# The opening of an attention stage: centroid norms in a chain of their own, similarities by thirds, another order around the second head

## The chip, the cores and the metric

The kernel runs on one core of one Trainium2 chip. The metric is the device time of one launch, in microseconds (us). A core has a matrix engine (TensorE, PE in the profile, with its weight loads as PEld), a vector engine (VectorE, DVE), a scalar engine (ScalarE, ACT), a general engine (GpSimd, POOL) and a sync engine (SyncE, SP) that here only issues DMA transfers. Each engine takes its own instructions strictly in the order in which they are written, and waits on semaphores for the others. ACT can issue DMA transfers as well; they then have their own queue.

## What is computed

An attention with clusters, followed by two expert layers. Only the attention's opening is touched.

```python
q_n = q / (np.linalg.norm(q, axis=-1, keepdims=True) + 1e-06)
k_n = k / (np.linalg.norm(k, axis=-1, keepdims=True) + 1e-06)
c_n = centroids / (np.linalg.norm(centroids, axis=-1, keepdims=True) + 1e-06)
q_assign = np.argmax(np.einsum('bhsd,hcd->bhsc', q_n, c_n), axis=-1)
k_assign = np.argmax(np.einsum('bhsd,hcd->bhsc', k_n, c_n), axis=-1)
mask = q_assign[:, :, :, None] == k_assign[:, :, None, :]
scores = np.where(mask, scale * np.matmul(q, k.transpose(0, 1, 3, 2)), -1000000000.0)
...
x = _moe_ref(x=x, **moe_kwargs)
return _moe2_ref(x=x, **moe2_kwargs)
```

There are 2 batches and 8 heads, so 16 pairs of batch and head (called heads here), each with 768 tokens of 64 numbers, and 16 centroids a head. The first expert layer norms its 8 expert embeddings of 512 numbers (`en = expert_emb / norm`) and divides by a number tau; the kernel folds those embeddings into a small matrix while attention still opens.

## The kernel before

A head's queries and keys come as six tiles each of 128 tokens. PE transposes the 12 tiles in three groups of four (`transpose_raw`): tiles 0 to 3 are queries, 4 and 5 queries and 6 and 7 keys, 8 to 11 keys. Every group is then split into a high part by ACT (`prep` stages 0, 1 and 2, semaphore `prep_hi`) and a low part by DVE (the same stages, semaphore `prep_lo`, one count for each group, so that the first head's groups are 1 to 3 and the second head's 4 to 6). `similarities` multiplies the 12 tiles with the 16 centroids of the head, two matmuls of 16 columns for a tile (L369 and L370 for queries, L372 and L373 for keys). DVE takes the maximum over the 16 and turns it into a cluster number (`prep` stage 4: L665, L667, L638, L676); the keys' numbers go into a small tile (`attn_key_id_b`, L770), PE spreads them over all partitions (`key_ids`, L379), and ACT copies that out (L559, semaphore `kid_ready`).

Attention itself goes by query tiles n = 0, 1, 2 and so on. PE makes `scores` (four matmuls of 384 columns, L417 and L418), DVE compares cluster numbers (`mask`, L685) and adds the mask while it takes the row maximum (`maxima`, L697, semaphore `max_done`), ACT makes the exponentials (L564), PE transposes them (L428), ACT and DVE split the transposed tile (L570 and L643, `attn_probs_t_hi` and `attn_probs_t_lo`), PE multiplies with the values (L447). `step(0)` is the first step of the regular pipeline, in which scores run three tiles ahead. Two score banks are used in turn, so `scores(2)` needs the maximum of tile 0 taken.

Ahead of that pipeline stands an opening that is written out by hand, engine by engine, and it is this that the change rewrites:

- `UnitRows` norms the centroids (128 rows of 64) and the expert embeddings (8 rows of 512) together. DVE squares and sums both, ACT takes one square root over both columns (L149), DVE refines it with six small operations (`newton`) and writes the unit centroids (L169, two operations); the unit embeddings are written much later (L169 again), just ahead of the first mask.
- PE transposes the unit centroids (L504), ACT (L608, L609) and DVE (L643 on `attn_c_lo` and `attn_c_hi_over_lo`) split them.
- `warm(n)` issues n matmuls of 512 columns on constants whose result nobody reads; `WARM` holds their numbers, in the order in which they are called.
- PE transposes the 8 heads' unit embeddings (L525, semaphore `experts_t`); DVE scales them by 1/tau into `fold` (L784, semaphore `x_done`), ahead of its third `maxima`.

ACT needs a table for square roots and another for exponentials, and loads one when it changes (ACT_TABLE_LOAD).

## Time and profile before

| what | us |
|---|---|
| median of 3 runs | 1592.2 |
| lowest and highest of them | 1591.24 and 1592.25 |
| the profiled execution, its own time | 1594.29 |
| its span, first to last instruction | 1592.5 |
| PE busy in it | 1568.3 (98%) |
| DVE busy | 1190.0 (75%) |
| ACT busy | 770.6 (48%) |

The views used are the page (engines' busy time, the chain of waits), the timeline of the opening (each row one instruction or a run of like ones, with the idle time ahead of it and what ended that) and windows (busy time of each engine in a stretch, the clock granted to TensorE as a share of full, the DMA engines' share and rate). Attention takes about the first 480 us of the span, and its opening the first 25 us.

### The profile page before, as it was taken

The page shows a single profiled execution, that of the slowest core. Times are in us where ns is not written, and L with a number is a line of the kernel's source. Part 1 is how long each engine was busy: PE and PEld are TensorE (multiplying, and loading weights), DVE is VectorE, ACT ScalarE, POOL GpSimd, SP SyncE. Part 2 cuts the span into 40 slices and gives each one's busy share as a digit, 9 for nine tenths or more (in the row PEclk, how much of TensorE's full clock was granted, in tenths as well). Part 3 has the DMA queues.
Part 4 walks back from the last instruction along what each step waited for, and adds up shares of the span by engine and source line. Part 5 has one row for each costly group of instructions (what it writes and reads, how often), then busy time and mean ns, then how long its engine had stood idle before and what let it go on. Part 6 is the DMA issues. An engine that isn't in the chain of part 4 may idle for free.

```text
span 1592.5 us, 27473 instructions
## 1 busy us (share of the span) xinstructions
PE 1568.3 (98%) x8404; PEld 1390.7 (87%) x8404; DVE 1190.0 (75%) x2026; ACT 770.6 (48%) x1418; POOL 263.7 (17%) x343
## 2 busy tenths in 40 slices
PE   8999999999999999999999999999999999999998
PEld 7999999778888788989999898989899998989897
DVE  7999999999999976876656666666656566666664
ACT  5777779888888852323232323233232333232321
POOL 2111111342333550000100100010001001100102
PEclk9999999999999999999999999999999999999999
DMA  4222323354344310100110010011001100100002
GB/s 101 61 60 69 79 59 90 86 198 148 143 151 151 106 41 27 40 28 27 47 33 27 29 51 27 27 40 40 27 27 45 35 27 28 52 26 27 27 0 79
DMA packets 123701, 94.92 MB, mean 60 GB/s; under 512 B 66345, under 2 KB 101161, under 8 KB 123633
## 3 DMA queue, kind: packets, MB, share of 16 engines
q1 hardware_dynamic: 120848, 86.01, 17.8%
q0 software_dynamic: 2480, 8.13, 1.5%
q8 instruction: 21, 0.34, 0.1%
q14 instruction: 48, 0.39, 0.1%
q10 hardware_dynamic: 304, 0.05, 0.0%
HBM read 87.88 MB, written 6.29 MB: 59 GB/s over the span
## 4 chain that ended last, share of the span: by engine, by line
PE 88%; DVE 7%; issue 3%; ACT 2%; DVEq 0%; DMA 0%; ACTq 0%; POOL 0%
PE moe_bank L1381 11%; PE moe_bank L1383 11%; PE moe_bank L1382 11%; PE moe_bank L1356 10%; PE moe_bank L1359 10%; PE moe_bank L1358 10%; PE attn_ps_out L447 3%; PE attn_ps_probs_t L428 2%; PE moe_bank L1316 2%; PE moe_bank L1318 2%; PE moe_bank L1317 2%; PE moe_bank L1299 2%; PE moe_bank L1301 2%; PE moe_bank L1300 2%; DVE attn_scores L697 1%
## 5 line engine op out<-in xcount | busy, mean ns | idle before, releaser
L2035 DVE SCALAR_TENSOR_TENSOR all_x<-moe_bank,all_x 128x512 f32<-128x512 f32 x336 | 251.4, 749 | 130.8 <-PE moe_bank L1383 130.2
L1356 PE MATMUL moe_bank<-moe_x_t_hi,all_w_hi 128*128 128x384 f32 x896 | 303.0, 338 | 2.0 <-DVE all_w_lo L889 1.4
L1359 PE MATMUL moe_bank<-moe_x_t_hi,all_w_lo 128*128 128x384 f32 x896 | 302.5, 338 | 0.0
L1381 PE MATMUL moe_bank<-moe_w_hi,moe_h_hi 128*128 128x512 f32 x768 | 302.3, 394 | 0.0
L1358 PE MATMUL moe_bank<-moe_x_t_lo,all_w_hi 128*128 128x384 f32 x896 | 301.1, 336 | 0.0
L1382 PE MATMUL moe_bank<-moe_w_lo,moe_h_hi 128*128 128x512 f32 x768 | 300.5, 391 | 0.0
L1383 PE MATMUL moe_bank<-moe_w_hi,moe_h_lo 128*128 128x512 f32 x672 | 264.5, 394 | 0.0
L1356 PEld LDWEIGHTS moe_bank<-moe_x_t_hi,all_w_hi 128*128 128x128 f32 x896 | 168.4, 188 | 13.4 <-issue 2.0
L1358 PEld LDWEIGHTS moe_bank<-moe_x_t_lo,all_w_hi 128*128 128x128 f32 x896 | 168.4, 188 | 10.0
L1359 PEld LDWEIGHTS moe_bank<-moe_x_t_hi,all_w_lo 128*128 128x128 f32 x896 | 168.2, 188 | 0.0
L2196 POOL TENSOR_TENSOR moe_w_sums<-moe_dense_w_raw 128x256 f32<-128x256 f32 x32 | 24.8, 774 | 842.4 <-DVE all_w_lo L889 842.4
L1382 PEld LDWEIGHTS moe_bank<-moe_w_lo,moe_h_hi 128*128 128x128 f32 x768 | 144.1, 188 | 23.0
L1381 PEld LDWEIGHTS moe_bank<-moe_w_hi,moe_h_hi 128*128 128x128 f32 x768 | 144.3, 188 | 21.5
L1383 PEld LDWEIGHTS moe_bank<-moe_w_hi,moe_h_lo 128*128 128x128 f32 x672 | 126.0, 188 | 30.1
L1729 ACT ACTIVATE moe_h_hi<-all_x 128x384 fp32r<-128x384 f32 x63 | 33.1, 525 | 170.4 <-DVE all_x L2147 170.4
L889 DVE TENSOR_TENSOR moe_routed_w_lo<-moe_w_raw,moe_routed_w_hi 128x1024 fp32r<-128x1024 f32 x76 | 112.8, 1524 | 0.1
L1705 ACT ACTIVATE moe_h_hi<-moe_p 128x384 fp32r<-128x384 f32 x63 | 33.1, 525 | 143.2 <-DVE moe_p L2101 143.2
L2101 DVE TENSOR_TENSOR moe_p<-moe_bank,moe_p 128x384 f32<-128x384 f32 x63 | 35.1, 557 | 86.8 <-PE moe_bank L1359 76.1
L643 DVE TENSOR_TENSOR attn_probs_t_lo<-attn_ps_probs_t,attn_probs_t_hi 128x384 fp32r<-128x384 f32 x192 | 97.3, 547 | 2.4 <-ACT attn_probs_t_hi L570 1.3
L1724 ACT ACTIVATE moe_h_hi<-moe_bank 128x384 fp32r<-128x384 f32 x63 | 31.0, 492 | 134.2 <-PE moe_bank L1359 134.2
L697 DVE CUSTOM_DVE_ANT_0 attn_scores<-attn_ps_scores,attn_mask 128x768 f32<-128x768 f32 x96 | 91.2, 950 | 2.5 <-issue 0.6
L564 ACT ACTIVATE attn_probs<-attn_scores,attn_row_max 128x768 f32<-128x768 f32 x96 | 91.4, 952 | 3.4 <-DVE attn_row_max L697 3.3
(339 smaller groups left out, 3071.4 us busy)
## 6 DMA issues: line engine op xcount, KB each, us to landing
all_w_raw<-in_moe_w SPq DMA_DIRECT2D x8, 2048.0 KB, 7.5
moe_w_raw<-in_moe_w SPq DMA_DIRECT2D x8, 2048.0 KB, 8.3
moe_dense_w_raw<-in_moe_w SPq DMA_DIRECT2D x64, 256.0 KB, 2.9
moe_dense_w_raw<-in_moe_w SPq DMA_DIRECT2D x32, 512.0 KB, 3.4
attn_q_raw<-in_q SPq DMA_DIRECT2D x32, 192.0 KB, 3.0
attn_k_raw<-in_k SPq DMA_DIRECT2D x32, 192.0 KB, 3.5
attn_v_raw<-in_v SPq DMA_DIRECT2D x16, 192.0 KB, 3.5
tokens<-all_x SPq DMA_DIRECT2D x32, 96.0 KB, 1.9
```

Of the source, the lines that this page charges most:

```text
L447: mm = pe.matmul(out, V2[j][:, m, :], probs[(s0 // 3) % 2][:, m, :], start=(m == 0 and probs is PTH), stop=(m == T - 1 and probs is PTL))
L564: act.activation(PR[s % 2][:], SM[s % 2][:], ACT.Exp, bias=MX[s % 2][:], scale=-1.0, accum_out=SUM[:, s % 12:s % 12 + 1]).then_inc(exp_don ...
L643: return dve.tensor_tensor(out, src, hi.bitcast(F32), ALU.subtract)
L697: dve.tensor_tensor_reduce(out=SM[s % 2][:].rearrange("p (a k) -> p a k", a=2), in0=ps_s[s % 2][:, :, 0:3 * P], in1=MASK[s % 2][:].rearran ...
L889: return dve.tensor_tensor(out, src, hi.bitcast(F32), ALU.subtract)
L1356: pe.matmul(out, hi[:, s, k, :], XH[chunk][:, x, k, :], start=(start and k == 0), stop=False, skip_group_check=True)
L1358: pe.matmul(out, hi[:, s, k, :], XL[chunk][:, x, k, :], start=False, stop=False, skip_group_check=True)
L1359: mm = pe.matmul(out, lo[:, s, k, :], XH[chunk][:, x, k, :], start=False, stop=(stop and k == 1), skip_group_check=True)
L1381: pe.matmul(out, HH[h][hidden][:, rows], W2H[j][:, f, :], start=(f == 0), stop=False)
L1382: pe.matmul(out, HH[h][hidden][:, rows], W2L[j][:, f, :], start=False, stop=False)
L1383: mm = pe.matmul(out, HL[h][hidden][:, rows], W2H[j][:, f, :], start=False, stop=(f == 1))
L2035: dve.scalar_tensor_tensor(acc, y, PROB[:, row, bass.ds(at, 1)], acc, ALU.mult, ALU.add).then_inc(y_added, 1)
```

## The change

The two norms become two chains. The centroids' chain has its own load (from ACT's queue, as before), sum, root, refinement and write. The embeddings' chain is loaded from SP's queue, its squares are summed by ACT (one activation that also sums), its root is taken by ACT later, its refinement is done by DVE right ahead of the first head's maxima over similarities, and ACT instead of DVE writes the unit embeddings. The first head's keys are loaded from ACT's queue, right behind the centroids, instead of from SP's; tau is loaded from SP's queue behind the second head's transfers. PE transposes the unit centroids ahead of the first keys, and ACT and DVE split them ahead of the second group. The 24 similarity matmuls of the first head come in three groups of 8, each waiting only for its own low part. `scores(0)` and four more matmuls of `warm` go ahead of the second head's transposes; the second head's last group of tiles goes behind the keys' numbers on PE and ACT, and behind the second `maxima` on DVE; `scores(2)` goes ahead of the second head's similarities and the embeddings' transposes.

```diff
-WARM = (8, 4, 6)
+WARM = (8, 4, 4, 6)
...
+        dve.tensor_reduce(self.s[0], self.square[:], AX.X, ALU.add).then_inc(self.summed, 1)
+
+    def sums_of_squares(self, act):
+        act.wait_ge(self.loaded, 16)
+        act.activation(self.square[:], self.raw[:], ACT.Square, accum_out=self.s[0]).then_inc(self.summed, 1)
 
     def roots(self, act):
-        act.wait_ge(self.step, self.SUMS)
-        act.activation(self.s[:, 1, :], self.s[:, 0, :], ACT.Sqrt).then_inc(self.root, 1)
+        act.wait_ge(self.summed, 1)
+        act.activation(self.s[1], self.s[0], ACT.Sqrt).then_inc(self.root, 1)
 
     def scale(self, dve):
-        s, step = self.s, self.step
-        dve.memset(s[:], 1.0).then_inc(step, 1)
-        for j, (rows, _) in enumerate(self.arrays):
-            raw, square = self.raw[j], self.square[j]
-            dve.wait_ge(self.loaded[j], 16)
-            dve.tensor_tensor(square[:], raw[:], raw[:], ALU.mult).then_inc(step, 1)
-            dve.wait_ge(step, 2 + 2 * j)
-            dve.tensor_reduce(s[0:rows.shape[0], 0, j:j + 1], square[:], AX.X, ALU.add).then_inc(step, 1)
         dve.wait_ge(self.root, 1)
-
-        newton(dve, step, self.SUMS, s[:, 0, :], s[:, 1, :], s[:, 2, :], s[:, 3, :])
-        dve.wait_ge(step, self.SUMS + 6)
-
-    def write(self, dve, j):
-        rows, outs = self.arrays[j]
-        for out in outs:
-            raw = self.raw[j][:].rearrange("r (h d) -> r h d", d=DH) if len(out.shape) == 3 else self.raw[j][:]
-            dve.tensor_scalar(out, raw, self.s[0:rows.shape[0], 2, j:j + 1], None, ALU.mult).then_inc(self.step, 1)
+        newton(dve, self.step, 0, *self.s)
+
+    def outputs(self):
+        for out in self.outs:
+            yield out, self.raw[:].rearrange("r (h d) -> r h d", d=DH) if len(out.shape) == 3 else self.raw[:]
+
+    def write(self, dve):
+        dve.wait_ge(self.step, self.SCALED)
+        for out, raw in self.outputs():
+            dve.tensor_scalar(out, raw, self.s[2], None, ALU.mult).then_inc(self.written, 1)
+
+    def write_by_scalar(self, act):
+        act.wait_ge(self.step, self.SCALED)
+        for out, raw in self.outputs():
+            act.activation(out, raw, ACT.Copy, scale=self.s[2]).then_inc(self.written, 1)
...
+        cents = UnitRows(mem, "centroids", centroids.rearrange("h c d -> (h c) d"), [unit[:, 0], unit[:, 1]])
+        embeddings = UnitRows(mem, "embeddings", expert_emb, [unit_experts[:, :, 0, :], unit_experts[:, :, 1, :]])
...
             for half in range(2):
                 sp.dma_start(QR[0][:, :, half, :], qd[0:1].rearrange("o p t d -> p (o t) d")).then_inc(first_q, 16)
-            for half in range(2):
-                sp.dma_start(KR[0][:, :, half, :], kd[0:1].rearrange("o p t d -> p (o t) d")).then_inc(first_k, 16)
             sp.dma_start(VR[0][:], vd[0:1].rearrange("o p t d -> p (o t) d")).then_inc(first_v, 16)
+            embeddings.load(sp)
             load(1, 1)
+            sp.dma_start(TAU[:, 0:1], tau.rearrange("(o n) -> o n", o=1).broadcast_to([P, 1])).then_inc(tau_loaded, 16)
             load_next(2, 0)
             load_next(3, 1)
...
-                    warm(WARM[2], ps_o[:])
+                    warm(WARM[3], ps_o[:])
...
             pe.wait_ge(first_q, 32)
             transpose_raw(0, 0, 4).then_inc(prep_ready, 1)
             transpose_raw(0, 4, 2, ps_t[:, 0], 4)
+            pe.wait_ge(cents.written, 2)
+            pe.transpose(ps_o[:, 0:P], unit[:].rearrange("p o d -> p (o d)"), c["ident"][:]).then_inc(cent_ready, 1)
             pe.wait_ge(first_k, 32)
             transpose_raw(0, 6, 2, ps_t[:, 0], 4).then_inc(prep_ready, 1)
             transpose_raw(0, 8, 4, ps_t[:, 1]).then_inc(prep_ready, 1)
-            pe.wait_ge(rows.step, rows.FIRST)
-            pe.transpose(ps_o[:, 0:P], unit[:].rearrange("p o d -> p (o d)"), c["ident"][:]).then_inc(cent_ready, 1)
             warm(WARM[1])
             pe.wait_ge(cent_split, 4)
-            pe.wait_ge(prep_lo, 3)
-            similarities(0, 0, ps_o[:, P:P + 2 * T * NC], 0)
-            similarities(0, 0, ps_o[:, P:P + 2 * T * NC], T).then_inc(prep_ready, 1)
+            for first in range(0, 2 * T, 4):
+                pe.wait_ge(prep_lo, first // 4 + 1)
+                mm = similarities(0, 0, ps_o[:, P:P + 2 * T * NC], first, 4)
+            mm.then_inc(prep_ready, 1)
+            scores(0, 0, 0)
+            warm(WARM[2], ps_s[1][:, 1])
             pe.wait_ge(raw_loaded[1], LOADS)
             transpose_raw(1, 0, 4, ps_s[1][:, 0]).then_inc(prep_ready, 1)
             transpose_raw(1, 4, 4, ps_s[1][:, 1]).then_inc(prep_ready, 1)
-            transpose_raw(1, 8, 4, ps_t[:, 1]).then_inc(prep_ready, 1)
-            scores(0, 0, 0)
             pe.wait_ge(idb_ready, 1)
             key_ids(ps_t[:, 0], 0)
             key_ids(ps_p[:], 3)
+            transpose_raw(1, 8, 4, ps_t[:, 1]).then_inc(prep_ready, 1)
             pe.wait_ge(prep_lo, 5)
             scores(1, 1, 0)
+            pe.wait_ge(max_done, 1)
+            scores(2, 2, 0)
             pe.wait_ge(kid_ready, 2)
             pe.wait_ge(prep_lo, 6)
             similarities(1, 1, ps_p[:], 0)
-            pe.wait_ge(rows.step, rows.DONE)
+            pe.wait_ge(embeddings.written, 2)
             for h in range(H):
                 mm = pe.transpose(ps_o[:, h * E:(h + 1) * E], unit_experts[:, h].rearrange("e o d -> e (o d)"),
                                   c["ident"][0:E, 0:E])
             mm.then_inc(experts_t, 1)
-            pe.wait_ge(max_done, 1)
-            scores(2, 2, 0)
...
-            rows.load(act)
-            act.dma_start(TAU[:, 0:1], tau.rearrange("(o n) -> o n", o=1).broadcast_to([P, 1])).then_inc(tau_loaded, 16)
-            rows.roots(act)
-            act.wait_ge(made, 4)
-            act.activation(TABLE[:], c["rank16"][:, 0:1], ACT.Exp)
+            cents.load(act)
+            for half in range(2):
+                act.dma_start(KR[0][:, :, half, :], kd[0:1].rearrange("o p t d -> p (o t) d")).then_inc(first_k, 16)
+            cents.roots(act)
             prep(0, 0, 0)
-            prep(0, 0, 1, ps_t[:, 0])
-            prep(0, 0, 2, ps_t[:, 1])
             act.wait_ge(cent_ready, 1)
             act.activation(CH[:], ps_o[:, 0:P], ACT.Copy).then_inc(cent_split, 1)
             act.activation(CHL[:], ps_o[:, 0:P], ACT.Copy).then_inc(cent_split, 1)
+            prep(0, 0, 1, ps_t[:, 0])
+            prep(0, 0, 2, ps_t[:, 1])
+            embeddings.sums_of_squares(act)
+            embeddings.roots(act)
+            act.wait_ge(made, 4)
+            act.activation(TABLE[:], c["rank16"][:, 0:1], ACT.Exp)
+            embeddings.write_by_scalar(act)
             prep(1, 1, 0, ps_s[1][:, 0], 5)
             prep(1, 1, 1, ps_s[1][:, 1], 6)
-            prep(1, 1, 2, ps_t[:, 1], 7)
-            prep(0, 0, 5, ps_t[:, 0], 8)
-            prep(0, 0, 6, ps_p, 9)
+            prep(0, 0, 5, ps_t[:, 0], 7)
+            prep(0, 0, 6, ps_p, 8)
+            prep(1, 1, 2, ps_t[:, 1], 9)
...
-            rows.scale(dve)
-            rows.write(dve, 0)
+            cents.sums(dve)
+            cents.scale(dve)
+            cents.write(dve)
             prep(0, 0, 0)
-            prep(0, 0, 1, ps_t[:, 0])
-            prep(0, 0, 2, ps_t[:, 1])
             dve.wait_ge(cent_split, 2)
             low(CL[:], ps_o[:, 0:P], CH[:]).then_inc(cent_split, 1)
             low(CHL[DH:P, :], ps_o[DH:P, 0:P], CH[DH:P, :]).then_inc(cent_split, 1)
+            prep(0, 0, 1, ps_t[:, 0])
+            prep(0, 0, 2, ps_t[:, 1])
             dve.wait_ge(made, ALL_MADE)
+            embeddings.scale(dve)
             prep(0, 0, 4, ps_o[:, P:P + 2 * T * NC])
             dve.wait_ge(ids_step, 3)
             dve.tensor_copy(IDB[:], ID[0][:, T:2 * T]).then_inc(idb_ready, 1)
             prep(1, 1, 0, ps_s[1][:, 0])
             prep(1, 1, 1, ps_s[1][:, 1])
-            prep(1, 1, 2, ps_t[:, 1])
-            rows.write(dve, 1)
             mask(0, 0, 0)
             maxima(0, 0)
             mask(1, 1, 0)
             maxima(1, 1)
+            prep(1, 1, 2, ps_t[:, 1])
             mask(2, 2, 0)
```

What stands in a row on three engines, before and after; `attn_qk_hi1` and `attn_q_lo1` are the second head's split tiles, with 64x512 the last group.

DVE around the first mask, before:

```order
L655 SCALAR_TENSOR_TENSOR attn_qk_hi1<-attn_ps_scores1,attn_qk_hi1 64x256
L655 SCALAR_TENSOR_TENSOR attn_qk_hi1<-attn_ps_probs_t,attn_qk_hi1 64x512 [waits attn_prep_hi]
L169 TENSOR_SCALAR attn_unit_experts<-attn_raw1,attn_row_norms 8x8x64 x2
L685 TENSOR_SCALAR attn_mask0<-attn_key_id_rows0,attn_cluster_id0 128x768 [waits attn_kid_ready]
L697 ISA attn_scores0,attn_row_max0<-attn_ps_scores0,attn_mask0 128x768 [waits attn_scores_ready,attn_mask_ready]
L697 ISA attn_row_max0 128x1
L685 TENSOR_SCALAR attn_mask1<-attn_key_id_rows0,attn_cluster_id0 128x768
```

and after:

```order
L668 SCALAR_TENSOR_TENSOR attn_qk_hi1<-attn_ps_scores1,attn_qk_hi1 64x256
L698 TENSOR_SCALAR attn_mask0<-attn_key_id_rows0,attn_cluster_id0 128x768 [waits attn_kid_ready]
L710 ISA attn_scores0,attn_row_max0<-attn_ps_scores0,attn_mask0 128x768 [waits attn_scores_ready,attn_mask_ready]
L710 ISA attn_row_max0 128x1
L698 TENSOR_SCALAR attn_mask1<-attn_key_id_rows0,attn_cluster_id0 128x768
L710 ISA attn_scores1,attn_row_max1<-attn_ps_scores1,attn_mask1 128x768 [waits attn_scores_ready,attn_mask_ready]
L710 ISA attn_row_max1 128x1
L668 SCALAR_TENSOR_TENSOR attn_qk_hi1<-attn_ps_probs_t,attn_qk_hi1 64x512 [waits attn_prep_hi]
```

The last group (64x512) moved from ahead of the first mask to behind the second maxima, and the two writes of unit experts left this engine.

PE from the second head's first transposes on, before:

```order
L343 MATMUL attn_ps_scores1<-all_ident,attn_q_raw1 128x128 [waits attn_raw_loaded1]
L343 MATMUL attn_ps_scores1<-all_ident,attn_q_raw1 128x128 x5
L343 MATMUL attn_ps_scores1<-all_ident,attn_k_raw1 128x128 x2
L343 MATMUL attn_ps_probs_t<-all_ident,attn_k_raw1 128x128 x4
L417 MATMUL attn_ps_scores0<-attn_qk_hi0 128x384
L418 MATMUL attn_ps_scores0<-attn_qk_hi0,attn_q_lo0 128x384
L417 MATMUL attn_ps_scores0<-attn_qk_hi0 128x384
L418 MATMUL attn_ps_scores0<-attn_qk_hi0,attn_q_lo0 128x384
L379 MATMUL attn_ps_probs_t<-all_identb,attn_key_id_b 128x128 [waits attn_key_id_b_ready]
L379 MATMUL attn_ps_probs_t<-all_identb,attn_key_id_b 128x128 x2
L379 MATMUL attn_ps_prep<-all_identb,attn_key_id_b 128x128 x3
```

and after, from the first head's scores:

```order
L424 MATMUL attn_ps_scores0<-attn_qk_hi0 128x384
L425 MATMUL attn_ps_scores0<-attn_qk_hi0,attn_q_lo0 128x384
L424 MATMUL attn_ps_scores0<-attn_qk_hi0 128x384
L425 MATMUL attn_ps_scores0<-attn_qk_hi0,attn_q_lo0 128x384
L499 MATMUL attn_ps_scores1<-all_onesb 128x512 x4
L350 MATMUL attn_ps_scores1<-all_ident,attn_q_raw1 128x128 [waits attn_raw_loaded1]
L350 MATMUL attn_ps_scores1<-all_ident,attn_q_raw1 128x128 x5
L350 MATMUL attn_ps_scores1<-all_ident,attn_k_raw1 128x128 x2
L386 MATMUL attn_ps_probs_t<-all_identb,attn_key_id_b 128x128 [waits attn_key_id_b_ready]
L386 MATMUL attn_ps_probs_t<-all_identb,attn_key_id_b 128x128 x2
L386 MATMUL attn_ps_prep<-all_identb,attn_key_id_b 128x128 x3
L350 MATMUL attn_ps_probs_t<-all_ident,attn_k_raw1 128x128 x4
```

Scores of tile 0 and four constant matmuls now stand ahead of the second head's transposes, and the last four of these behind the keys' numbers.

ACT from its first instructions, before:

```order
L145 DMA attn_raw0<-in_centroids 128x64
L145 DMA attn_raw1<-in_moe_expert_emb 8x512
L600 DMA attn_tau<-in_moe_tau 128x1
L149 ACT_TABLE_LOAD
L149 ACTIVATE attn_row_norms<-attn_row_norms 128x2 [waits attn_rows_step]
L603 ACT_TABLE_LOAD
L603 ACTIVATE attn_exp_of_rank<-all_rank16 128x1 [waits all_const_made]
L549 ACTIVATE attn_qk_hi0<-attn_ps_prep 128x512 [waits attn_prep_ready]
L549 ACTIVATE attn_qk_hi0<-attn_ps_probs_t 128x256 [waits attn_prep_ready]
```

and after:

```order
L144 DMA attn_centroids_raw<-in_centroids 128x64
L610 DMA attn_k_raw0<-in_k 128x6x64 x2
L158 ACT_TABLE_LOAD
L158 ACTIVATE attn_centroids_norms<-attn_centroids_norms 128x1 [waits attn_centroids_summed]
L558 ACTIVATE attn_qk_hi0<-attn_ps_prep 128x512 [waits attn_prep_ready]
L614 ACTIVATE attn_c_hi<-attn_ps_out 128x128 [waits attn_cent_ready]
L615 ACTIVATE attn_c_hi_over_lo<-attn_ps_out 128x128
L558 ACTIVATE attn_qk_hi0<-attn_ps_probs_t 128x256 [waits attn_prep_ready]
L560 ACTIVATE attn_qk_hi0<-attn_ps_probs_t 128x256
L560 ACTIVATE attn_qk_hi0<-attn_ps_probs_t 128x512 [waits attn_prep_ready]
```

The second table load moved behind the first head's copies and two embeddings operations, and the first head's keys are issued ahead of the first table load.

## Rows read from the trace of the kernel before

**Rows 1.** The page: the chain that ended last by engine.

```profile
PE 88%; DVE 7%; issue 3%; ACT 2%; DVEq 0%; DMA 0%; ACTq 0%; POOL 0%
```

**Rows 2.** Windows, regular attention: us from and to, length, busy us (count), clock, DMA, GB/s.

```profile
30.00:60.00 30.00, 29.66 (x210) 27.90 (x209) 29.66 (x73) 24.25 (x57) 3.23 (x5) 1.00 0.30 73
```

**Rows 3.** Timeline, transfers of the opening: start, length, engine, what.

```profile
1.22 0.78 ACTq L145 DMA_DIRECT2D attn_raw<-in_moe_expert_emb  x1
...
2.21 1.33 SPq L318 DMA_DIRECT2D attn_k_raw<-in_k  x2
...
5.35 1.28 ACT L603 ACT_TABLE_LOAD   x1
...
5.47 0.63 PE L343 MATMUL attn_ps_prep<-all_ident,attn_q_raw 128*128 128x128 f32 x4 [0.86 <-POOL all_fold L123]
...
6.72 0.87 PE L343 MATMUL attn_ps_probs_t<-all_ident,attn_k_raw 128*128 128x128 f32 x6 [0.40 <-DMA attn_k_raw<-in_k]
6.75 0.58 ACT L549 ACTIVATE attn_qk_hi<-attn_ps_prep 128x512 fp32r<-128x512 f32 x1
...
7.51 1.15 SPq L293 DMA_DIRECT2D attn_v_raw<-in_v  x1
```

**Rows 4.** Timeline, ACT and DVE: root and end of the centroids' chain, then the splitting.

```profile
5.13 0.20 ACT L149 ACTIVATE attn_row_norms<-attn_row_norms 128x2 f32<-128x2 f32 x1 [1.43 <-DVE attn_row_norms L159]
...
6.57 0.42 DVE L169 TENSOR_SCALAR attn_unit_centroids<-attn_raw,attn_row_norms 128x64 f32<-128x64 f32 x2
...
7.37 0.69 DVE L643 TENSOR_TENSOR attn_q_lo<-attn_ps_prep,attn_qk_hi 128x512 fp32r<-128x512 f32 x1 [0.38 <-ACT attn_qk_hi L549]
...
8.40 1.03 DVE L655 SCALAR_TENSOR_TENSOR attn_qk_hi<-attn_ps_probs_t,attn_qk_hi 64x256 fp32r<-64x256 f32 x2
...
9.79 0.29 DVE L643 TENSOR_TENSOR attn_c_hi_over_lo<-attn_ps_out,attn_c_hi 64x128 fp32r<-64x128 f32 x1
```

**Rows 5.** Timeline, PE: constant matmuls, the second head's transposes, scores of tile 0.

```profile
7.54 1.03 PE L492 MATMUL attn_ps_scores<-all_onesb 128*128 128x512 bf16 x4
...
14.55 1.54 PE L343 MATMUL attn_ps_scores<-all_ident,attn_q_raw 128*128 128x128 f32 x6
...
17.49 0.49 PE L418 MATMUL attn_ps_scores<-attn_qk_hi,attn_q_lo 128*128 128x384 f32 x1
...
17.81 0.34 PE L417 MATMUL attn_ps_scores<-attn_qk_hi 128*128 128x384 f32 x1
```

**Rows 6.** Windows over the opening (columns as in Rows 2), from two answers.

```profile
4.00:6.00 2.00, 1.14 (x8) 0.57 (x7) 1.59 (x6) 0.85 (x2) 1.37 (x6) 1.00 1.12 239
...
8.57:10.14 1.57, 0.00 (x0) 0.00 (x0) 1.45 (x4) 0.13 (x1) 0.30 (x1) 1.00 1.11 251
10.14:10.90 0.76, 0.76 (x7) 0.76 (x7) 0.00 (x0) 0.00 (x0) 0.00 (x0) 1.00 0.62 162
10.90:14.54 3.64, 3.64 (x19) 3.64 (x18) 0.00 (x0) 0.00 (x0) 0.00 (x0) 0.51 1.05 236
```

**Rows 7.** Timeline, DVE and ACT from the first head's maxima to the first mask.

```profile
14.81 0.36 DVE L665 TENSOR_REDUCE attn_sim_max<-attn_ps_out 128x12 f32<-128x192 f32 x1 [4.72 <-PE attn_ps_out L373]
...
18.04 0.69 DVE L655 SCALAR_TENSOR_TENSOR attn_qk_hi<-attn_ps_probs_t,attn_qk_hi 64x512 fp32r<-64x512 f32 x1
...
18.76 0.87 DVE L169 TENSOR_SCALAR attn_unit_experts<-attn_raw,attn_row_norms 8x512 f32<-8x512 f32 x2
...
18.93 0.48 ACT L559 ACTIVATE attn_key_id_rows<-attn_ps_prep 128x384 bf16<-128x384 f32 x1
...
19.56 0.40 DVE L685 TENSOR_SCALAR attn_mask<-attn_key_id_rows,attn_cluster_id 128x768 bf16<-128x768 bf16 x1
```

**Rows 8.** Timeline: what stands between the first mask and regular attention.

```profile
20.91 0.66 PE L525 MATMUL attn_ps_out<-all_ident,attn_unit_experts 8*128 8x8 f32 x8
...
23.44 0.96 DVE L697 CUSTOM_DVE_ANT_0 attn_scores<-attn_ps_scores,attn_mask 128x768 f32<-128x768 f32 x1
...
25.35 0.92 PE L428 MATMUL attn_ps_probs_t<-all_ident,attn_probs 128*128 128x128 f32 x6 [0.30 <-DVE attn_probs_t_lo L643]
```

34 lines of the change are left out of this document (17 added, 17 removed).

## The prediction, made before the changed kernel ran

> **What bounds the kernel now.** I read the page's chain first: 88% of it is PE's work, 7% DVE's [rows 1]. In regular attention PE and DVE are both busy 29.66 of 30 us [rows 2]; neither has room to make good a late start, so what the opening gains or loses reaches the end one for one. The change touches nothing behind the opening. The question is then how much earlier PE enters the regular pipeline. A good mark is PE's second transposes of probabilities, 25.35 in the trace: they waited for DVE's low parts, which follow the third row maximum, started at 23.44 [rows 8]. The time of that third maximum is my meter: everything behind it is the same in both kernels.
>
> Then I read the opening in order of time. PE transposes the first head's queries at 5.47 and the keys at 6.72, each when their transfers have landed [rows 3]. DVE gets its first high part only at 7.37, since ACT was loading its exponential table (5.35, 1.28 long) and copied at 6.75 [rows 3, 4]. DVE then works without a break to 10.1, the centroids' parts last [rows 4]; PE does nothing from 8.57 to 10.14 [rows 6]. Its 24 similarity matmuls run to 14.7: the first 7 at the full level of the clock (0.76 us for 7, 0.11 each), the other 17 at half of it, 1.2 GHz (clock 0.51, 3.64 us for 17, 0.21 each) [rows 6]. DVE's maximum starts at 14.81, its first mask at 19.56 [rows 7].
>
> **Up to the similarities: 3.5 us earlier.** ACT now issues two key transfers ahead of its square root table. A pair cost SP 1.33 [rows 3]; from 1.22 on that ends at 2.6, the table load of 1.28 at 3.9, and the root no longer waits for the embeddings (it stood at 5.13). From root to unit centroids it is 6.99 less 5.13, 1.86 [rows 4], so they are ready at 5.8, under the query transposes; these end at 6.3, then the centroids' transpose takes 0.1. The exponential table is out of the way: ACT copies at 6.1 instead of 6.75, DVE starts at 6.75 instead of 7.37. Its five splitting operations still take 2.7 together, but the two for the centroids are second and third: done by 8.0. PE has the keys at 6.72 as before (taken unchanged: the DMA engines are full from 4 to 6 us, share 1.12 [rows 6], so an earlier issue brings little; if it brought the whole 1.0 us the following would be 0.4 us earlier, the bound on that side). Its six transposes end at 7.4, four constant matmuls take 1.0 [rows 5], and at 8.4 instead of 10.14 the first third starts: 1.75 gained. A third is 8 x 0.11 = 0.9; second and third start at 9.3 and 10.2, when their low parts (8.9 and 9.5) are there. The splitting by thirds therefore costs no wait, and PE's own work is the bound. They end near 11.2, with or without a fall of the clock at 10.9 as in the trace. DVE can start at 11.3 instead of 14.81: 3.5 earlier.
>
> The embeddings' six refinement steps stand ahead of that maximum on DVE. Six such steps took 1.2 (5.37 to 6.57, the latter in [rows 4]); DVE is free for them at 9.5, so they end at 10.7, covered by the third third of the similarities; without that cover they would cost 1.2. ACT's square with sum (near 0.7, as its 512 wide copy of 0.58 and an accumulator read), root 0.2, table 1.28 and two writes (0.5 each) lie between 8.1 and 11.8, ahead of the second head's first copy near 13.4: free. Loading tau and the embeddings from SP moves the second head's transfers by 0.6 us at most either way, and v's last one, issued at 7.51 before, lands by 12.0 if it takes the 4.5 us that the first keys took from 2.21 to 6.72 [rows 3]; PE asks at 12.2 or later: free.
>
> **From there to the first mask: 4.1 or 2.6 us earlier.** PE now does scores of tile 0 and four constant matmuls before the second head's transposes. At the full level that is 0.7 + 1.0, and these transposes start at 12.8; at the half level (0.32 for each scores matmul [rows 5], and some 1.7, between 1.0 and 2.0, for the constants) at 14.15; before, at 14.55 [rows 5]. Transposes of the first four tiles 0.65, ACT's three copies 1.03 (an estimate: 0.58 for 512 columns [rows 3] and two of 256 that overlap), its two copies of the keys' numbers 0.38 and 0.49 [rows 7] give 2.6 to the mask with the hops: 15.4 or 16.9, instead of 19.56. Before it was 5.0, as DVE did a last split (0.69) and the unit experts (0.87) ahead of the mask [rows 7]. The keys' numbers are at hand: DVE made them in 1.7 from its maximum, so by 13.0.
>
> **From the first mask to the third maximum: 2.2 us lost.** Before, that was 23.44 less 19.56, 3.9. Now DVE takes mask (0.40) and maximum (0.96) twice, with hops of 0.2 between them (3.0 up to the end of the second), then the split that was moved there (0.69): 3.7. PE stands behind it with the second head's similarities (it waits for that low part), 12 x 0.11 = 1.35, and the embeddings' transposes, 0.66 [rows 8]: 5.7. Only then can DVE write the fold matrix (0.3), and its third maximum is queued behind that: 6.1 instead of 3.9. Behind PE's wait stand the first transposes of probabilities and scores of tile 3. So a stall goes and a new one comes: PE has nothing for 1.4 us after scores of tile 2.
>
> **Sum.** Third maximum at 15.4 + 6.1 = 21.5 (full level) or 23.0 (half level) instead of 23.44: 1.9 or 0.4 us earlier. Nothing says how other executions fall between these levels, so I take the middle, -1.0. The profiled execution was 1594.29 with a span of 1592.5; its likes would be 1593.3 and 1591.5. The median of the runs shown lies 2.1 below the profiled one, 1592.2, and becomes **1591.2**. Taking the bounds of the terms (keys 0.4 earlier; constants dearer by 0.3) this case alone reaches from 1589.5 to 1592.3.
>
> **Rival 1, slower: the clock falls in the new wait.** Before the fall at 10.9, PE had done nothing for 1.57 us and then only 16 column matmuls [rows 6]. The change takes that stretch away but makes another: from the end of scores of tile 2 (mask + 2.4) 1.4 us of nothing, 1.35 us of 16 column matmuls, 0.66 us of 8 column ones. Its likeness speaks for a fall there. Against: the same embeddings' transposes, behind the same similarities but without the idle time, still took 0.66 for eight in the trace [rows 8], at the full level. Price: at half level the next six transposes cost 0.6 more, scores of tile 3 another 0.6, the 12 key similarities 1.25 (0.21 less 0.11 each), and if it lasts over the following step another 1 to 2: 2.5 to 5. I take 3.9 on top of -1.0: +2.9, **1595.1**. It decides from the point at which the fall costs more than the 1.0 gained, which is as soon as it reaches scores of tile 3.
>
> **Rival 2: queries and keys share the DMA engines.** The trace has both on one queue, the queries first, engines full. If two queues take turns, the four transfers of 128 x 384 numbers (0.197 MB each) at 239 GB/s [rows 6] are one stream of 3.3 us, and the queries land near its end, with the keys, 0.8 to 1.1 later than now. PE then has 0.4 more to do after the keys' arrival (the queries' last transposes), as DVE and ACT have slack up to 8.4: -0.6, **1591.6**. If the keys slip too, 1592.1. The Trainium skill states such a rule, in "DMA: Bandwidth & Descriptors", Queues, rings and completion order: each engine goes round robin between the queues it has work for. No row here shows two large transfers on two queues at once.
>
> **Rival 3, faster: the loss behind the mask doesn't come.** If the embeddings' transposes aren't last there (because PE comes to them with time to spare), the 2.2 shrinks to 0.7, the moved split alone: 1592.2 less 3.4 = **1588.8**. Against it stands the written order on PE, so little is left for it. That the thirds or the new order don't act at all is excluded: the order of each engine shows them.
>
> A rule on tables that speaks against this change: "ScalarE: Activation LUTs", What ACT_TABLE_LOAD costs, in the Trainium skill, gives 1.28 us for a load and 1.38 for a drain. By it, the root would come at 5.3 instead of 3.9, the unit centroids at 7.1, and all after it near 0.3 later. The trace disagrees: a load of 1.28 at 5.35 and the next copy of data at 6.75, with a small activation in between [rows 3]. The sum goes by the trace.
>
> **Chances.** Forecast 0.50, rival 1 0.25, rival 2 0.15, rival 3 0.10. A measurement of this kernel can tell about 0.2%, 3.2 us, from no change. Faster by more: rival 3 and a sliver of the forecast, 0.12. Slower by more: nearly half of rival 1 and a little else, 0.14. Within: 0.74. The range leaves out rival 3 and the upper part of rival 1, and takes in 1 us by which runs of one kernel differ: 1588.9 to 1595.9.
>
> **What would show it.** In the changed kernel's timeline: unit centroids before 6; the first similarities near 8.4, all 24 in under 3 us; DVE's first maximum over similarities near 11.3; the first mask between 15.4 and 17; then PE idle until DVE's last split, the fold behind the embeddings' transposes, and the third row maximum about 6.1 behind the first mask. Rival 1 shows as a clock of 0.5 somewhere between 20 and 30 us, rival 2 as query transposes near 6.3, rival 3 as a third maximum within 4.6 of the mask. I am wrong if the second head's transfers, not PE, set the start of its transposes, or if ACT's table or embeddings work runs into the second head's first copy.

## The result, and the profile after

The changed kernel takes 1602.28 us (median of 6 runs, 1598.81 to 1603.0), the kernel before 1592.22 (6 runs). The ratio is 1.0059, with an interval of 1.0046 to 1.0071: it is slower by about 0.6%. I had forecast 1591.2, with 1588.9 to 1595.9 as the range, and slower by over 0.2% at 0.14. That was wrong. The profiled executions lie 7.5 us apart (1601.79 against 1594.29), and 7.1 of those 7.5 can be followed in the opening. The difference of the medians is 10.1, since the profiled execution of before was 2.1 above its own median and that of the changed kernel 0.5 below.

From the page of the changed kernel:

```profile
span 1600.0 us, 27487 instructions
...
PE 1574.1 (98%) x8408; PEld 1393.2 (87%) x8408; DVE 1190.7 (74%) x2027; ACT 773.3 (48%) x1423; POOL 263.5 (16%) x343
...
PE 83%; DVE 9%; issue 5%; ACT 1%; DVEq 1%; DMA 1%; ACTq 0%; POOL 0%
```

The last line is that of [rows 1]: PE's share of the chain fell from 88% to 83%. The timeline of the changed kernel, up to the first mask (start, length, engine, what, and in brackets the idle time ahead and what ended it):

```profile
1.22 1.32 ACTq L610 DMA_DIRECT2D attn_k_raw<-in_k  x2
...
2.58 1.28 ACT L158 ACT_TABLE_LOAD   x1 [2.45 <-issue]
...
3.31 1.24 SPq L300 DMA_DIRECT2D attn_q_raw<-in_q  x2
...
3.87 0.20 ACT L158 ACTIVATE attn_centroids_norms<-attn_centroids_norms 128x1 f32<-128x1 f32 x1
...
6.19 0.63 PE L350 MATMUL attn_ps_prep<-all_ident,attn_q_raw 128*128 128x128 f32 x4 [1.54 <-DMA attn_q_raw<-in_q]
...
7.73 1.54 PE L350 MATMUL attn_ps_probs_t<-all_ident,attn_k_raw 128*128 128x128 f32 x6 [0.58 <-DMA attn_k_raw<-in_k]
...
9.06 1.91 PE L499 MATMUL attn_ps_scores<-all_onesb 128*128 128x512 bf16 x4
...
13.70 0.36 DVE L678 TENSOR_REDUCE attn_sim_max<-attn_ps_out 128x12 f32<-128x192 f32 x1 [1.79 <-PE attn_ps_out L380]
...
19.39 0.42 DVE L698 TENSOR_SCALAR attn_mask<-attn_key_id_rows,attn_cluster_id 128x768 bf16<-128x768 bf16 x1
```

The keys are issued at 1.22 instead of 2.21, and land a whole microsecond later: PE waits for the queries until 6.19 and for the keys until 7.73, where it was 5.47 and 6.72 [rows 3]. (The row at 5.47 puts that wait down to a copy on POOL; the kernel waits there only for constants that were ready long before, and for the queries.) On SP's queue everything behind the queries moved up into the keys' old place: the first head's values are issued at 2.22 instead of 3.59, the second head's queries at 3.31 instead of 4.85. The first maximum over similarities comes at 13.70, 1.1 us sooner than the 14.81 of [rows 7], not 3.5. The first mask comes at 19.39, against 19.56. From there on:

```profile
23.33 0.25 PE L376 MATMUL attn_ps_prep<-attn_c_hi_over_lo,attn_qk_hi 128*128 128x16 f32 x1 [1.33 <-DVE attn_qk_hi L668]
...
24.74 1.02 PE L536 MATMUL attn_ps_out<-all_ident,attn_unit_experts 8*128 8x8 f32 x8
...
25.68 1.54 PE L435 MATMUL attn_ps_probs_t<-all_ident,attn_probs 128*128 128x128 f32 x6
25.87 0.28 DVE L798 TENSOR_SCALAR all_fold<-attn_ps_out,attn_tau 128x64 f32<-128x64 f32 x1 [2.17 <-PE attn_ps_out L536]
26.29 0.96 DVE L710 CUSTOM_DVE_ANT_0 attn_scores<-attn_ps_scores,attn_mask 128x768 f32<-128x768 f32 x1
...
30.72 1.54 PE L435 MATMUL attn_ps_probs_t<-all_ident,attn_probs 128*128 128x128 f32 x6
...
33.34 2.27 PE L499 MATMUL attn_ps_out<-all_onesb 128*128 128x512 bf16 x6
...
38.06 0.82 PE L435 MATMUL attn_ps_probs_t<-all_ident,attn_probs 128*128 128x128 f32 x6
```

and the last of these in the kernel before:

```profile
30.96 0.82 PE L428 MATMUL attn_ps_probs_t<-all_ident,attn_probs 128*128 128x128 f32 x6
```

PE has nothing for 1.33 us until DVE's last low part is done (23.33), and DVE nothing for 2.17 us until the embeddings' transposes are. The third row maximum starts at 26.29 (23.44 before) and the second transposes of probabilities at 30.72 (25.35 before, [rows 8]): 5.4 us late. By the fourth, at 38.06 against 30.96, it is 7.1, and the next two (40.91 and 43.76 against 33.82 and 36.68) are 7.1 late as well. The remaining 0.4 of the profiled executions comes somewhere later and was not followed. Windows of the changed kernel (us from and to, length, busy us of PE, PEld, DVE, ACT and POOL with counts, clock, DMA share, GB/s):

```profile
7.50:10.90 3.40, 3.17 (x12) 2.19 (x12) 2.69 (x7) 2.50 (x9) 1.23 (x2) 0.52 1.30 222
...
14.30:17.70 3.40, 3.40 (x15) 2.41 (x15) 1.16 (x5) 0.60 (x1) 0.00 (x0) 0.53 0.42 97
...
24.60:28.00 3.40, 3.40 (x20) 3.35 (x21) 2.00 (x6) 1.23 (x3) 0.00 (x0) 0.52 0.00 0
28.00:31.40 3.40, 3.40 (x17) 3.40 (x16) 0.98 (x4) 0.67 (x2) 0.00 (x0) 0.50 0.00 0
31.40:34.80 3.40, 3.40 (x13) 2.26 (x12) 3.37 (x8) 1.91 (x4) 2.22 (x7) 0.50 0.01 2
34.80:38.00 3.20, 3.06 (x24) 2.16 (x22) 1.75 (x6) 2.19 (x5) 1.38 (x2) 0.98 0.07 15
```

The clock (third number from the end) was at half, 1.2 GHz, in five of these stretches: 7.5 to 10.9, 14.3 to 17.7, and without a break from 24.6 to 34.8. Before, it was at half only from 10.9 to 17.7, at the similarities and the second head's transposes (0.51 and 0.50 there, 0.98 or more in every stretch up to 38). So both rivals that I had kept apart came together: late transfers in the first 8 us, and a clock that falls behind the new wait.

### The profile page after: what moved, and what is told of

The parts are those of the page before. It is cut to its first block, busy times and chain, and to the rows that moved or that the text cites. A ratio compares the mean times of both kernels' runs of the same rounds, so it can differ in the third digit from the quotient of the medians.

```text
span 1600.0 us, 27487 instructions
## 1 busy us (share of the span) xinstructions
PE 1574.1 (98%) x8408; PEld 1393.2 (87%) x8408; DVE 1190.7 (74%) x2027; ACT 773.3 (48%) x1423; POOL 263.5 (16%) x343
## 3 DMA queue, kind: packets, MB, share of 16 engines
q1 hardware_dynamic: 119440, 85.64, 17.8%
## 4 chain that ended last, share of the span: by engine, by line
PE 83%; DVE 9%; issue 5%; ACT 1%; DVEq 1%; DMA 1%; ACTq 0%; POOL 0%
PE moe_bank L1395 11%; PE moe_bank L1397 11%; PE moe_bank L1396 11%; PE moe_bank L1370 10%; PE moe_bank L1373 10%; PE moe_bank L1372 10%; DVE attn_probs_t_lo L656 2%; PE moe_bank L1330 2%; DVE attn_scores L710 2%; PE moe_bank L1332 2%; PE moe_bank L1331 2%; PE moe_bank L1313 2%; PE moe_bank L1315 2%; PE moe_bank L1314 2%; PE attn_ps_out L454 2%
## 5 line engine op out<-in xcount | busy, mean ns | idle before, releaser
L1395 PEld LDWEIGHTS moe_bank<-moe_w_hi,moe_h_hi 128*128 128x128 f32 x768 | 144.3, 188 | 21.5
L579 ACT ACTIVATE attn_probs_t_hi<-attn_ps_probs_t 128x384 fp32r<-128x384 f32 x192 | 84.2, 495 | 19.5 <-PE attn_ps_probs_t L435 19.1
```

The lines of the kernel that those rows point to most:

```text
L579: act.activation(PTH[(s // 3) % 2][:, 3 * half:3 * half + 3, (s % 3) * P:(s % 3 + 1) * P], ps_t[:, half, 0:3 * P].rearrange("p (m s) -> p ...
L1395: pe.matmul(out, HH[h][hidden][:, rows], W2H[j][:, f, :], start=(f == 0), stop=False)
```

## The experiments

Each edit is against the changed kernel unless it says otherwise. "Fourth transposes" below are PE's fourth transposes of probabilities: 30.96 before, 38.06 in the changed kernel; by then a kernel is in its regular pipeline. Kernels that were measured together share the runs of the kernel before. In the twelve profiled executions, what the fourth transposes are late or early against the kernel before comes back in the time of the launch to within 0.8 us.

### Constant matmuls in the new wait

```diff
             scores(2, 2, 0)
+            warm(6, ps_o[:])
             pe.wait_ge(kid_ready, 2)
```

> The changed kernel with 6 more constant matmuls of 512 columns on PE, behind scores of tile 2 and ahead of the wait for the second head's last low part. They fill the 1.3 us in which PE had nothing (21.9 to 23.3 in the trace of after). Theory 1, the clock: the 7 us of loss at the first repeats of the regular pipeline come from TensorE's clock, which fell to half at 24.6 and stayed there to 34.8 after that idle stretch. With it kept up, the wait itself remains: third row maximum near 25.9, PE's second transposes of probabilities near 28.0 instead of 30.7, and nothing lost behind them, so some 2.7 us over the kernel before: 1595. Theory 2, the wait alone (what stands behind DVE's late split is late, whatever the clock): the time stays at 1602, since the wait is as long as it was, and the constant matmuls can only add up to 0.3.

Measured: 1597.12 (1595.74 to 1597.55), ratio 1.0025 (1.0016 to 1.0035), 5.2 less than the changed kernel and 2 above the 1595 of theory 1. Rows of the timeline of gap_warm, PE:

```profile
21.86 1.47 PE L499 MATMUL attn_ps_out<-all_onesb 128*128 128x512 bf16 x6
...
28.03 0.87 PE L435 MATMUL attn_ps_probs_t<-all_ident,attn_probs 128*128 128x128 f32 x6
```

Windows of the same kernel, over the two stretches that were at half before (columns as above):

```profile
24.60:28.00 3.40, 3.40 (x33) 3.36 (x32) 2.32 (x6) 1.90 (x4) 0.00 (x0) 1.00 0.00 0
28.00:31.40 3.40, 3.33 (x23) 2.32 (x23) 3.32 (x10) 2.18 (x5) 1.57 (x3) 1.00 0.01 2
```

Up to the wait all is as in the changed kernel (first mask 19.41, similarities of the second head at 23.36). Then the clock stays up and the second transposes start at 28.03, as theory 1 had it, the fourth at 33.59. Work that computes nothing, put where PE had nothing to do, gives back 4.5 of the 7.1 us (38.06 less 33.59). The wait alone costs less than its consequence. What is left, 2.6, is the lateness that reached the second transposes.

### Keys from SP's queue again

```diff
+            for half in range(2):
+                sp.dma_start(KR[0][:, :, half, :], kd[0:1].rearrange("o p t d -> p (o t) d")).then_inc(first_k, 16)
             sp.dma_start(VR[0][:], vd[0:1].rearrange("o p t d -> p (o t) d")).then_inc(first_v, 16)
             embeddings.load(sp)
...
             cents.load(act)
-            for half in range(2):
-                act.dma_start(KR[0][:, :, half, :], kd[0:1].rearrange("o p t d -> p (o t) d")).then_inc(first_k, 16)
```

> The changed kernel with the first head's keys loaded from SP's queue again, behind the queries (v, embeddings, the rest behind them). Theory 1, shared DMA engines: two queues made both late; now queries are transposed at 5.5 instead of 6.2 and keys at 6.7 instead of 7.7, the clock stays at full from 7.5 to 10.9, the first similarities start near 8.4 instead of 10.4, and the first mask comes at 15.4 to 17 instead of 19.4. The total gains 2 to 4 us on the changed kernel if the clock behind the mask goes as before, and is 1597 to 1600; by the clock it can also fall elsewhere. Theory 2, the transfers are bound by bandwidth whoever issues them: keys at 7.7 as now, and the total stays at 1602.

Measured: 1599.89 (4 runs, 1595.3 to 1601.21), ratio 1.0044 (1.0027 to 1.006). The timeline of keys_sp:

```profile
5.31 0.67 PE L352 MATMUL attn_ps_prep<-all_ident,attn_q_raw 128*128 128x128 f32 x4 [0.39 <-DMA attn_q_raw<-in_q]
...
6.93 0.88 PE L352 MATMUL attn_ps_probs_t<-all_ident,attn_k_raw 128*128 128x128 f32 x6 [0.62 <-DMA attn_k_raw<-in_k]
...
8.32 0.36 PE L378 MATMUL attn_ps_out<-attn_c_hi_over_lo,attn_qk_hi 128*128 128x16 f32 x1
...
11.28 0.36 DVE L678 TENSOR_REDUCE attn_sim_max<-attn_ps_out 128x12 f32<-128x192 f32 x1 [0.63 <-PE attn_ps_out L382]
...
16.81 0.42 DVE L698 TENSOR_SCALAR attn_mask<-attn_key_id_rows,attn_cluster_id 128x768 bf16<-128x768 bf16 x1
```

Windows of the same kernel (columns as above), where the changed kernel first fell, and ahead of the embeddings:

```profile
7.50:10.90 3.40, 3.40 (x30) 3.01 (x28) 2.67 (x11) 3.34 (x9) 1.51 (x2) 1.00 1.09 228
21.20:24.60 3.40, 3.40 (x26) 3.35 (x26) 1.38 (x4) 0.61 (x2) 0.00 (x0) 0.69 0.02 5
```

Queries and keys are there at 5.31 and 6.93, the similarities start at 8.32, DVE's maximum at 11.28 and the first mask at 16.81. These are the prediction's numbers (8.4, 11.3, and 16.9 at the half level). Theory 1 holds: in these two executions the second queue cost 2.6 us at the first mask, 0.8 of it as later keys and most of the rest through the clock, which was at half from 7.5 on in one and not in the other. But behind the mask the clock fell again, now without the late transfers; so that fall has its own cause. It was at full up to 22.4, at half from 23.0 to 25.5 and at full again from 26.0, behind a wait of 1.34 us like the changed kernel's 1.33. So the same wait can be followed by a long fall or by a short one. This execution, at 1595.3, is the fastest of the four; the others took 1598.95 to 1601.21, and of them no trace was taken.

### DVE's last split one place sooner

```diff
             maxima(0, 0)
+            prep(1, 1, 2, ps_t[:, 1])
             mask(1, 1, 0)
             maxima(1, 1)
-            prep(1, 1, 2, ps_t[:, 1])
```

> The changed kernel with one move on DVE: the second head's last low part behind the first row maximum instead of behind the second. PE's similarities of the second head then wait for nothing once scores of tile 2 are out (21.9), the embeddings' transposes end near 23.9, and the third row maximum starts near 24.5 instead of 26.3. Theory 1 (the idle stretch let the clock fall): with the stretch gone the clock stays at full from 24.6 to 34.8 and the second transposes of probabilities start near 26.6 instead of 30.7: 1593.5 to 1594. Theory 2 (wait alone): 1.8 us less than the changed kernel, 1600.

Measured: 1596.03 (1594.69 to 1600.25), ratio 1.0024 (1.0013 to 1.0034). The timeline of split_early:

```profile
21.40 0.25 PE L376 MATMUL attn_ps_prep<-attn_c_hi_over_lo,attn_qk_hi 128*128 128x16 f32 x1
...
23.40 1.54 PE L435 MATMUL attn_ps_probs_t<-all_ident,attn_probs 128*128 128x128 f32 x6
```

A window of the same kernel (columns as above):

```profile
24.60:28.00 3.40, 3.40 (x21) 3.40 (x20) 1.79 (x6) 1.63 (x4) 0.00 (x0) 0.68 0.00 0
```

The second head's similarities start at 21.40 instead of 23.33, and the first transposes of probabilities at 23.40 instead of 25.68, more than expected, as the first mask came 0.4 sooner in this execution. Theory 1 wanted the clock up afterwards. It was not in this execution: the transposes at 23.40 took 1.54 instead of the 0.82 of the full level, and the window from 24.6 on shows 0.68. Yet the fall was much shorter than the 10.2 us of the changed kernel (at full to 23.0, at full again from 27), with the fourth transposes at 33.22. The median, 6.3 below the changed kernel, is far more than the 1.8 of theory 2. So removing the wait took away most of the loss, but PE had no idle time between scores of tile 2 and this fall: the narrow matmuls can be followed by one without the wait.

### Both: keys from SP, constants in the wait

> Both edits: keys from SP's queue and 6 constant matmuls in the gap. If the two causes are separate, their gains add up: early part at the prediction's times (first mask 15.4 to 17), no fall of the clock behind it, third row maximum at mask plus 6.1, so 21.5 to 23.1, and the total 1590.5 to 1592, no slower than the kernel before. If only one of them is real, it comes out as the better of the two single edits, 1595 or above.

Measured: 1594.09 (1593.21 to 1595.54), ratio 1.0008 (0.9999 to 1.0018). First mask 17.18, fourth transposes 31.35. The gains add up: of the 7.1 us at the fourth transposes 4.5 go with the clock and 2.2 with the keys (33.59 less 31.35), and 0.4 is left. The medians say the same: 5.2 less by the constants alone, 2.4 by the keys alone, 8.2 by both. Where I expected 1590.5 to 1592 it is 2.1 to 3.6 above, so the rest of the change does not bring the 1.0 us forecast: by the medians it is 1.6 behind the kernel before, not clear of no change.

### Both: keys from SP, split sooner

> Both single edits that removed a cause: keys from SP's queue, and DVE's last low part of the second head behind the first row maximum. If PE's queue sets the entry into the regular pipeline (similarities of the second head, embeddings' transposes, then the first transposes of probabilities), then with the first mask at 16.8 to 17.2 the similarities start right behind scores of tile 2, near 19.3, the first transposes of probabilities near 21.5 and the second near 24.2, 1.1 ahead of the kernel before: 1591.3 with the clock at full, and 1593 to 1596 if it falls at 21.2 for one stretch as in the profile of keys_sp. The rival, that DVE's third row maximum sets it, gives that maximum at 22.0 and the same -1.4; the two part in the run with fold late.

Measured: 1594.16 (1592.64 to 1598.12), ratio 1.0015 (1.0004 to 1.0025). In the profiled execution (1592.64) the transposes of probabilities start at 21.50 and 24.17, as expected (21.5, 24.2), with the clock at full from 17.8 on. The opening can be 1.2 us ahead of the kernel before and the median still 0.9 behind it: 3 of the 10 runs took 1597.07 to 1598.12.

### The same without the added constants

```diff
-WARM = (8, 4, 4, 6)
+WARM = (8, 4, 0, 6)
```

> As keys_sp_split_early, without the four constant matmuls ahead of the second head's transposes. They took 1.7 us at half the clock (10.9 to 14.3 was at half in keys_sp). If PE's queue is the bound there, the second head's transposes start at 12.0 to 12.3 instead of 13.3 (the transfers have landed by then), the first mask near 15.6, and the total is 1.2 lower than keys_sp_split_early, 1590 if the clock is given back at 14.3 by the transposes alone. If the constants are what gives it back, the clock stays at half to 17.7, the transposes cost twice, and the total is 1.5 or more higher.

Measured: 1591.91 (1590.25 to 1594.92), ratio 0.9992 (0.9982 to 1.0001). Its timeline:

```profile
11.88 1.49 PE L352 MATMUL attn_ps_scores<-all_ident,attn_q_raw 128*128 128x128 f32 x6
...
15.42 0.42 DVE L698 TENSOR_SCALAR attn_mask<-attn_key_id_rows,attn_cluster_id 128x768 bf16<-128x768 bf16 x1
...
19.87 0.87 PE L437 MATMUL attn_ps_probs_t<-all_ident,attn_probs 128*128 128x128 f32 x6
```

The second head's transposes start at 11.88 instead of 13.51 and the first mask comes at 15.42 instead of 17.05: 1.6 us, the price, mostly at half the clock, of four matmuls that nobody reads. PE's real work alone brought the clock back (at half from 12.0 to 14.8, at full when the scores follow at 15.44; 19.87 took 0.87, the full level). The second transposes of probabilities start at 22.53, 2.8 ahead of the kernel before.

> The same kernel as keys_sp_split_early_nowarm, timed again in more rounds, since its interval against the kernel before touched 1. By PE's second transposes of probabilities (22.5 instead of 25.4) it should be up to 2.8 us faster than the kernel before; the first timing gave 1.3. If the gain is real and only blurred by stretches of half clock elsewhere, 1.5 to 3 us faster, with the interval clear of 1; if it was chance, within 0.7 of it.

Measured again with more runs: 1592.21 (1589.97 to 1594.64, 11 runs) against 1593.33, ratio 0.9993 (0.9984 to 1.0002). Two timings agree on 1.1 to 1.3 us, less than the 1.5 I asked for, and neither interval is clear of 1. The profile of this timing caught another execution of the same program: its first mask came at 15.30, but its transposes of probabilities at 19.84 took 1.54, at half the clock, and the next started at 23.97, 1.4 later than in the other one. From the first mask to those transposes the two executions of one program take 4.45 and 4.54 us; what follows differs by the clock. They are not alike in all: they ran on two chips, and the keys came at 6.78 in one and at 7.30 in the other.

### Two constants where PE was idle for 0.6 us

```diff
+            warm(2, ps_o[:])
             pe.wait_ge(max_done, 1)
             scores(2, 2, 0)
```

against keys_sp_split_early_nowarm.

> keys_sp_split_early_nowarm with two constant matmuls on PE ahead of its wait for the first row maximum, where it was idle for 0.6 us. If some of the executions of the kernel without them lose a stretch of half clock between 17 and 28 (its times spread from 1590.3 to 1594.9), they should spread less here and the median come out 0.5 to 1.5 lower; if the spread comes from elsewhere (the routing at 553 to 560, the end), both have the same median within 0.3.

Measured: 1591.94 (1590.06 to 1592.77, 11 runs), ratio 0.9991 (0.9982 to 1.0). The spread is 2.7 us instead of 4.7, the median only 0.3 lower. The first part of the expectation came out for the spread, the second for the median; eleven runs of each don't show that the spreads differ. Of its profiled execution:

```profile
14.78 0.42 DVE L699 TENSOR_SCALAR attn_mask<-attn_key_id_rows,attn_cluster_id 128x768 bf16<-128x768 bf16 x1
...
19.23 0.87 PE L437 MATMUL attn_ps_probs_t<-all_ident,attn_probs 128*128 128x128 f32 x6
```

This profile is no evidence for the two constants. From the mask to the transposes it takes 4.45 us, as without them, and its mask is 0.6 earlier because the clock was at full from 10.9 to 14.3 (0.60 in the other execution), ahead of the place of the edit. It is the lowest median of the study, 1.4 us under the kernel before, at the limit of what was measured.

### What sets the start of the regular pipeline: the fold matrix moved back

```diff
             mask(2, 2, 0)
+            step(0, 0)
             dve.wait_ge(tau_loaded, 16)
...
-            for s in range(14):
+            for s in range(1, 14):
                 step(0, s)
```

on DVE, against keys_sp_gap_warm.

> keys_sp_gap_warm with DVE's fold matrix (which waits for the embeddings' transposes) moved from ahead of the third row maximum to behind step 0. My prediction took DVE's third maximum, queued behind that wait, as what sets the start of the regular pipeline. If so, the maximum starts near 21.2 instead of 23.7 and the second transposes of probabilities near 24.5 instead of 25.8: 1592.8. The rival: PE's own queue sets it (similarities, embeddings' transposes, transposes of probabilities, scores, 12 key similarities, 2.67 us from first to second transposes of probabilities): then the maximum moves and those transposes stay at 25.8, and the total stays at 1594.1.

Measured: 1594.38 (1592.68 to 1597.51), ratio 1.0007 (0.9997 to 1.0017), as keys_sp_gap_warm. Its timeline, with the first mask, the third row maximum, and the two transposes:

```profile
18.76 0.42 DVE L699 TENSOR_SCALAR attn_mask<-attn_key_id_rows,attn_cluster_id 128x768 bf16<-128x768 bf16 x1
...
23.20 0.96 DVE L711 CUSTOM_DVE_ANT_0 attn_scores<-attn_ps_scores,attn_mask 128x768 f32<-128x768 f32 x1 [0.19 <-DVE attn_mask L699]
...
24.70 0.87 PE L437 MATMUL attn_ps_probs_t<-all_ident,attn_probs 128*128 128x128 f32 x6
...
27.36 0.88 PE L437 MATMUL attn_ps_probs_t<-all_ident,attn_probs 128*128 128x128 f32 x6
```

and the same four in keys_sp_gap_warm:

```profile
17.18 0.42 DVE L699 TENSOR_SCALAR attn_mask<-attn_key_id_rows,attn_cluster_id 128x768 bf16<-128x768 bf16 x1
...
23.11 0.88 PE L437 MATMUL attn_ps_probs_t<-all_ident,attn_probs 128*128 128x128 f32 x6
...
23.71 0.96 DVE L711 CUSTOM_DVE_ANT_0 attn_scores<-attn_ps_scores,attn_mask 128x768 f32<-128x768 f32 x1
...
25.78 0.87 PE L437 MATMUL attn_ps_probs_t<-all_ident,attn_probs 128*128 128x128 f32 x6
```

The two executions differ early on. In this one the queries came at 5.58 against 5.11, and the keys' six transposes at 7.11 took 1.54, the half level (0.87 at 7.03 in the other), though both load the keys from SP's queue; the first mask is 1.6 later for it. (The clock column of the windows shows 1.00 there; the durations tell.) So the distance from the first mask counts. The third row maximum comes at mask + 4.4 instead of mask + 6.5. The transposes of probabilities come at mask + 5.9 and + 8.6 in both. So starting DVE's third maximum 2.1 us sooner moved nothing on PE, and PE's own queue sets the start. The rival holds, and my meter was the wrong one.

### The kernel before, with the keys from ACT's queue

```diff
-            for half in range(2):
-                sp.dma_start(KR[0][:, :, half, :], kd[0:1].rearrange("o p t d -> p (o t) d")).then_inc(first_k, 16)
...
             rows.load(act)
+            for half in range(2):
+                act.dma_start(KR[0][:, :, half, :], kd[0:1].rearrange("o p t d -> p (o t) d")).then_inc(first_k, 16)
```

against the kernel before.

> The kernel before with one part of the change: the first head's keys from ACT's queue, behind centroids and embeddings. Theory 1 (two queues share the DMA engines): queries transposed near 6.2 instead of 5.47 and keys near 7.7 instead of 6.72, and the clock at half from 7.5 to 10.9. The first similarities start near 11.3 instead of 10.1; they then run at the full level to 14.0 instead of 14.7, so the total moves little, 0 to 1.2 us above the kernel before. Theory 2 (the lateness in the changed kernel comes from the centroids' transpose or from the embeddings' transfer ahead of them, not from the queue): queries at 5.4 and keys at 6.7 or sooner, the rest as before.

Measured: 1594.98 (1591.67 to 1596.23), ratio 1.0008 (0.9999 to 1.0018), 1.7 above the kernel before by medians, where at most 1.2 was expected. The timeline of before_keys_act:

```profile
5.68 0.63 PE L341 MATMUL attn_ps_prep<-all_ident,attn_q_raw 128*128 128x128 f32 x4 [0.92 <-DMA attn_q_raw<-in_q]
...
7.95 1.54 PE L341 MATMUL attn_ps_probs_t<-all_ident,attn_k_raw 128*128 128x128 f32 x6 [1.42 <-DMA attn_k_raw<-in_k]
...
14.51 0.36 DVE L665 TENSOR_REDUCE attn_sim_max<-attn_ps_out 128x12 f32<-128x192 f32 x1 [3.01 <-PE attn_ps_out L371]
...
22.50 1.49 PE L426 MATMUL attn_ps_probs_t<-all_ident,attn_probs 128*128 128x128 f32 x6
```

Windows of the same kernel (columns as above):

```profile
7.50:10.90 3.40, 2.95 (x11) 1.93 (x11) 2.18 (x5) 1.68 (x6) 0.71 (x1) 0.56 0.93 228
...
21.20:24.60 3.40, 3.40 (x16) 3.29 (x15) 3.13 (x9) 2.77 (x7) 0.00 (x0) 0.55 0.00 0
```

The keys come at 7.95, 1.2 us later than in the kernel before, and the clock is at half for most of 7.5 to 10.9 (0.56), in a kernel that has nothing else of the change. Theory 1 holds for the keys. The queries came only 0.2 later here, but that does not test how two queues share: the keys are issued at 2.03 here, behind the embeddings, and at 1.22 in the changed kernel, so they had less time beside the queries. Beside the keys stand the transfers that moved up on SP's queue (values at 2.21, the second head's queries at 2.88); how much of the lateness is theirs was not tested. That the embeddings' transfer on SP or the centroids' transpose made the keys late is excluded.

The second window shows something about the other cause. The kernel before has no wait behind the first mask, and here PE was busy without a gap from 19.24 on (12 matmuls of 16 columns, 8 of 8 columns, then scores), yet the clock fell at 21.5 and was back at 25. The keys' lateness had not reached that far: the first mask came at 19.23, 0.3 sooner than in the kernel before. The 0.9 us by which the fourth transposes were late (31.85) arose under that fall. So a fall behind these narrow matmuls does not need the new wait, and the kernel before is open to it too.

## Why the prediction was wrong

**The keys' arrival** was the first step that failed: "PE has the keys at 6.72 as before (taken unchanged...)", with an earlier arrival as the only bound. They came at 7.73. I had the mechanism as rival 2, and priced it at 0.4, with late queries only, and at 0.9 "if the keys slip too". Both were late, and the first mask lost 2.6. What the price left out is the clock: PE was idle for 1.54 and 0.58 us up to the keys, and the clock was at half from 7.5 on, so that the key transposes and four constant matmuls cost 3.2 us (7.73 to 10.9) instead of the 1.7 of the sum. That the idle time let it fall there fits keys_sp (0.39 and 0.62, and full) and before_keys_act (0.92 and 1.42, and half), but fold_late ran these transposes at half with 0.66 and no wait for the keys, so it is likely and not shown. The bound on the dear side was missing: with the engines already full [rows 6], another queue for the keys could only change the order in which transfers are served, and it let later ones (values, the second head's queries) be issued 1.4 and 1.5 us sooner, beside the keys. The prediction had allowed 0.6 at most for that. The keys were late in both kernels that issue them from ACT. The round robin that I cited from the Trainium skill ("DMA: Bandwidth & Descriptors", Queues, rings and completion order) fits that in direction; how evenly the queues took turns no run here shows. Late keys should have stood in the sum, with their price, and not beside it.

**Up to the first mask** the rest of the working was right. With the keys back on SP's queue, the first similarities (8.32), DVE's maximum (11.28) and the first mask (16.81) are the forecast 8.4, 11.3 and 16.9. But 16.9 is the case with the clock at half, and the sum took the middle between it and 15.4. Of the four profiled executions with the keys on SP's queue and the four added constants, three had the mask at 16.8 to 17.2 and fold_late at 18.76; none bore out the middle, which made the forecast 0.6 us too good. The embeddings' steps on DVE, ACT's work on the embeddings, the table load moved behind and tau's transfer cost nothing, as I had it. In the changed kernel the root's activation at 3.87 follows a load that started at 2.58 and took 1.28. The rule on the table's drain from the Trainium skill ("ScalarE: Activation LUTs", What ACT_TABLE_LOAD costs) is not borne out there.

**From the first mask to the third maximum** the sum was 6.1; measured, 6.5 with the clock at full, and 6.9 in the changed kernel. The term was right to a few tenths. That it is PE's queue (similarities, embeddings' transposes, then the transposes of probabilities) and not DVE's maximum that sets the start was wrong, and cost nothing in the number, since both come out of the same wait. It would have misled whoever acted on it: moving the fold matrix away from the maximum brings nothing.

**The clock behind the new wait** was the second step that failed, rival 1, at a chance of 0.25 and a price of 3.9. It came in the changed kernel's profiled execution and lasted 10.2 us, and cost 4.5 (gap_warm). In the profiled execution of keys_sp the same fall was short and cost 1.5 (the fourth transposes at 32.52 are 15.7 behind the first mask, with the constants added, 31.35, they are 14.2). The mechanism was named and its size was near, but not its weight: I gave it a quarter, since a like mix had once left the clock up. The place had 1.33 us of nothing and 2.0 of narrow matmuls; the stretch of the kernel before after which the clock fell at 10.9 had 1.57 and 0.8 [rows 6]. That likeness was the better evidence. The wait is not all of the cause: the clock fell without it in split_early, nowarm_again and before_keys_act, each time for less than half as long.

**The cases were added up as if they excluded each other.** Rivals 1 and 2 are separate causes, as the runs show: each edit alone leaves a loss (1597.12 and 1599.89), both together nearly none (1594.09). At the fourth transposes the runs give 0.4 for the rest of the change, where the sum had -1.0, 2.2 for the keys and 4.5 for the clock: the 7.1 seen there. The range ended at 1595.9 because no case in it had both; and with them my own prices, -1.0 + 0.9 + 3.9 on 1592.2, would have come to 1596.0. Rival 3 has a slip of its own: its 3.4 is 4.1 less 0.7, the case at the full clock, while the forecast takes the middle; by that it would have been near 1589.6 and not 1588.8.

What stays open: the median of the changed kernel lies 10.1 above that of the kernel before, the profiled execution 7.5. Of the other five executions no trace was taken. Their times stand in two groups, near 1598.9 and near 1602.8. That these differ in how long the clock stays down behind the wait fits the long fall of the changed kernel and the short one of keys_sp behind the same wait, but was not shown for this kernel. Why the fall lasted three times as long in one as in the other is open too.

## What to carry to other kernels

This opening, limited by transfers, was not made faster by issuing the keys from a second queue (7.73 and 7.95 instead of 6.72): look first at whether the DMA engines are already full, and at what moves up in the queue that the transfer leaves. And before work is moved so that TensorE waits once more, count what it does around that wait: here a wait of 1.33 us together with matmuls of a few columns was followed by a fall of the clock that cost 4.5, and six matmuls that compute nothing, placed exactly in the idle time, gave that back, while four ahead of real work cost 1.6. Where two mishaps have different causes, one of the cases must have both.

## What I had not expected of the hardware

Once fallen behind the wait, the clock stayed at half for 10.2 us (24.6 to 34.8) while PE was busy in every one of these microseconds by the profile (3.40 of 3.40 three times over): 16 column matmuls, transposes and scores at half speed did not bring it back in this execution, and it returned only during the six constant matmuls of 512 columns that follow (33.34, 2.27 us; the window from 34.8 on shows 0.98). In keys_sp, with the same order of work behind the mask, it was back at 26.0, among 16 column matmuls and ahead of any constants. And the same program finds the clock in different states at the same place: in two executions of keys_sp_split_early_nowarm, transposes of probabilities at 19.87 and at 19.84 took 0.87 and 1.54 us.
